# GpSimd's mixing steps spread over the quarters and tied to VectorE's steps, in a fused convolution with two expert layers

## The chip, the cores and the metric

The kernel runs on one core of one Trainium2 chip. The metric is the device time of one execution in microseconds; each version is run several times and the median is compared. Five engines of the core work here: PE (TensorE, matrix products, writes PSUM), DVE (VectorE), ACT (ScalarE), POOL (GpSimd, no access to PSUM) and SP (SyncE, which issues the DMAs). They are ordered against each other by semaphores only.

## The reference

`x` is 2 x 4096 x 192 (8192 tokens of 192 columns), everything in float32. Three parts follow each other.

```
w   = softmax(weight_gen, over k)                 # 7 weights per token and head, 8 heads of 24 columns
y0[s, h, :] = sum_k w[s, h, k] * x[s + k - 6, h, :]    # mixing over 7 tokens
u   = sigmoid(y0 @ w_gate) * (y0 @ w_val)         # 192 -> 1536
y   = u @ w_out1                                  # 1536 -> 192
h   = y @ w_in                                    # 192 -> 2048
g   = (a0 + a1 h + a2 h^2 + a3 h^3) / (1 + |b0| |h| + |b1| h^2 + 1e-6)
out = g @ w_out2                                  # 2048 -> 192
```

## The kernel before

The tokens are cut into 16 chunks of 512 (`NCH` = 16). Of the first layer a chunk has 12 units (128 of the 1536 columns each), of the second 16 (128 of the 2048). A loop over `k` of 73 steps, called quarters here, issues the work of every engine in an order written out by hand; a chunk of the first layer takes four quarters with three units each, and the second layer runs `OFF2` = 5 quarters behind with four units a quarter. In quarter `k`, `m = 3k`, `n = 4(k - 5)`, `p = n/2`.

PE's order within a quarter is the string `QUARTER`. "1" is `in1`: two products for a unit of the first layer (gate and value), each of them five matmuls (a float32 number is split into a high and a low part, so x and the weights come in parts). "2" is `in2`: one such product for a unit of the second layer. "a" and "b" are `out1` and `out2`: the unit's part in the layer's output, 8 matmul records each, added up in `acc1` and `acc2`. "a" lags one unit behind "1" (`A_LAG`), "b" eight units behind the quarter's first "2" (`B_LAG`). "X" transposes the mixed tokens of the next chunk (in the quarter with k % 4 = 3), "Y" transposes the first layer's output (k % 4 = 0). Products and transposes go into a ring of four PSUM banks; `wait_bank` makes PE wait until the bank used four places earlier is free: a gate product's by ACT's sigmoid, a value product's by `gated`, a "2" product's by `cubic`, a transpose's by `x_low` or `y_low`.

For a unit of the first layer ACT does `sigmoid` (L421) and DVE `gated` (L594). For a unit of the second ACT does `hidden` (L429, L430, L432: |b0 h|, h squared, a3 h + a2) and DVE `quadratic` (L601) and `cubic` (L607). These all read PSUM. For a pair of units DVE does `denominator` (L614); for four units ACT does `rsqrt` (L439) and `rsqrt_squared` (L446) on the denominator, which is a first estimate of its reciprocal; for a pair DVE does `newton_product` (L621), `reciprocal` (L628) and `quotient` (L637), after which "b" may run. These four DVE operations read two tensors in SBUF, 1024 elements a partition. Sigmoid and rsqrt need different tables of ACT, so there are two table loads a quarter.

A chunk's mixing is 13 steps (`mix`): a multiplication of the window by the weights of tap 0 into `mixed` (L519), then six times a multiplication into `prod` (L523) and an addition to `mixed` (L527). Chunk 0 is mixed by DVE, all others by GpSimd, which has nothing else to do: it begins a chunk when the transposes of the one before are done and its window is loaded, and runs through all 13 steps. `x_twice` (ACT, L396) then writes the last 64 columns a second time, since the transposes want 2 x 128 columns; `x_high` and `x_low` (ACT L404, L405; DVE L572, L575) split the transposed chunk. SP's order is `load_window(c)`, which waits for all 13 steps of chunk c - 1, and `store(c - 4)`. The first quarters also hold the softmax (L543 to L558) and the splitting of the weights (L564, L384).

Of the kernel before, what the change touches and what calls it, by code (L numbers as in the profile page):

```python
# [7 lines left out]
ALU = mybir.AluOpType  # L8
# [3 lines left out]
P = 128  # L12
T = 512
DA, DB = 128, 64
# [9 lines left out]
QUARTER = "12a212abbbXbYa12"  # L24
A_LAG = 1
B_LAG = 8
# [6 lines left out]
def moe_kernel(nc, x, weight_gen, w_gate, w_val, w_out1, w_in, w_out2, coef_a, coef_b, out):  # L33
# [34 lines left out]
    with ExitStack() as ctx:  # L68
        def sb(name, shape, dt=F32):
            return ctx.enter_context(nc.sbuf_tensor(name, shape, dt))  # L70
# [18 lines left out]

        window = sb("window", [P, WIN])  # L90
        mixw = sb("mixw", [P, CW])
        mixed = sb("mixed", [P, J, 2 * P])
# [3 lines left out]
        yt = [[sb(f"yt{b}_{n}", [P, T], F32R) for n in range(4)] for b in range(2)]  # L96
        ysb = sb("ysb", [P, J, 2 * P])
# [180 lines left out]
        def _(pe):  # L278
# [55 lines left out]
            def transposes(u, j, src):  # L334

                wait_bank(pe, u, j, 0)
                for n in range(J):
                    nc.tensor.transpose(bank(u, j, 0)[:, n * P:(n + 1) * P], src[:, n, 0:DA], ident[:, :])  # L338
                wait_bank(pe, u, j, 1)
                for n in range(J):  # L340
                    last = nc.tensor.transpose(bank(u, j, 1)[:, n * P:(n + 1) * P], src[:, n, DA:2 * P], ident[:, :])  # L341
                return last

            def x_transposes(j):
                pe.wait_ge(s_twice, j + 1)
                transposes("X", j, mixed).then_inc(s_xT, 1)

            def y_transposes(j):
                pe.wait_ge(s_ysb, j + 1)
                transposes("Y", j, ysb).then_inc(s_yT, 1)  # L350
# [29 lines left out]
        def _(act):  # L380
# [11 lines left out]
            def x_twice(j):  # L392
                if not 0 <= j < NCH:
                    return
                act.wait_ge(s_mix, MIXES * (j + 1))
                nc.scalar.copy(mixed[:, :, D:2 * P], mixed[:, :, DA:D]).then_inc(s_twice, 1)  # L396
# [77 lines left out]
            for k in range(NK):  # L474
                m, n, q = 3 * k, 4 * (k - OFF2), k - OFF2
                sigmoid(m)
                if k == 0:
                    split_high(4)
                    split_high(5)
                    exponential(1)  # L480
                    split_high(6)
                    split_high(7)
                hidden(n)
                if k % 4 == 0:
                    y_copy(k // 4 - 1)
                if k % 4 == 2:
                    x_twice((k + 1) // 4 + 1)
                hidden(n + 1)
                sigmoid(m + 1)
                if k == 1:  # L490
                    exponential(2)
                if k in (2, 3):
                    for c in range(3 * k + 2, 3 * k + 5):
                        split_high(c)
                rsqrt(q - 1)
                hidden(n + 2)
                rsqrt_squared(q - 1)
                if k % 4 == 3:
                    x_high(k // 4 + 1)
                if k % 4 == 0:  # L500
                    y_high(k // 4 - 1)
                sigmoid(m + 2)
                hidden(n + 3)
                if (k - OFF2) % 4 == 1:
                    z_copy((k - OFF2 - 1) // 4 - 1)

        def mix(eng, engine, c, k):
            base = MIXES * c
            m = (k + 1) // 2
            taken = window[:, m * D:m * D + J * D].rearrange("p (j h g) -> p j h g", h=H, g=G)  # L510
            total = mixed[:, :, 0:D]
            weights = softw[:, c * CW:(c + 1) * CW] if c < 2 else mixw[:, :]
            wk = weights.rearrange("p (j h k) -> p j h k", h=H, k=K)[:, :, :, m:m + 1].to_broadcast([P, J, H, G])
            if k == 0:
# [4 lines left out]
                engine.tensor_tensor(total.rearrange("p j (h g) -> p j h g", g=G), taken, wk,  # L519
                                     ALU.mult).then_inc(s_mix, 1)  # L520
            elif k % 2:
                wait(eng, s_mix, base + k if k > 1 else 0)
                engine.tensor_tensor(prod[:, :].rearrange("p (j h g) -> p j h g", h=H, g=G), taken, wk,  # L523
                                     ALU.mult).then_inc(s_mix, 1)
            else:
                eng.wait_ge(s_mix, base + k)
                engine.tensor_tensor(total, total, prod[:, :].rearrange("p (j d) -> p j d", d=D),  # L527
                                     ALU.add).then_inc(s_mix, 1)

        @block.vector  # L530
        def _(dve):
# [118 lines left out]
            for k in range(NK):  # L650
# [9 lines left out]
                quadratic(n)  # L660
                cubic(n)
                reciprocal(p - 3)
                denominator(p - 1)
# [12 lines left out]
                denominator(p)  # L676
                cubic(n + 1)
                quadratic(n + 2)
                cubic(n + 2)
                newton_product(p - 2)  # L680
                if k % 4 == 0:
                    y_low(k // 4 - 1)
                if k % 4 == 3:
                    x_low(k // 4 + 1)
                reciprocal(p - 2)
                gated(m + 2)
                quotient(p - 2)
                quadratic(n + 3)
                cubic(n + 3)
                newton_product(p - 1)  # L690

        @block.gpsimd
        def _(pool):
# [6 lines left out]
                                    base=0, pattern=[[-1, P]], channel_multiplier=1).then_inc(s_ident, 1)  # L700
            for c in range(1, NCH):
                for k in range(MIXES):
                    mix(pool, nc.gpsimd, c, k)
# [26 lines left out]
```

## Time and profile before

| | |
|---|---|
| median of 3 runs | 1509.95 us (1507.9 to 1510.64) |
| the profiled execution | 1511.6 us, of which the span of the trace is 1509.8 |
| mean granted clock of PE | 0.973 |
| PE busy | 1403.1 us, 93% of the span |
| DVE busy | 1277.7 us, 85% |
| ACT busy | 1047.7 us, 69% |
| GpSimd busy | 434.3 us, 29%, in 15 chunks |

All rows are of one profiled execution. A share is an average over three very different stages (the start, the steady quarters, the end without a first layer), so the stretches are read one by one. DVE's and PE's operations overlap a little at their ends: what one costs is read from start to start.

### The profile page before, as it was taken

Reading aid. Unit: us, or ns where it says so; the run is one execution under the profiler, and the core shown is the slowest. Engines: PE = TensorE matmul, PEld = TensorE weight load, DVE = VectorE, ACT = ScalarE, POOL = GpSimd, SP = SyncE. Lnnn points to the kernel's source line nnn. Section 1 sums busy time; section 2 is a strip of 40 time slices with the busy share of each in tenths; the row PEclk is TensorE's granted clock in tenths of the full one; section 3 lists DMA queues with packets and bytes.
Section 4 is the critical chain, followed back from the end, with each engine's and each line's share of the span. In section 5 each row is a group of like instructions: output and inputs, shape, how many; then the busy total and the mean of one; then the engine's idle time right before and its main releaser. Section 6 shows DMA issues by size and latency. Waiting matters only on the chain.

```text
span 1509.8 us, 18004 instructions
## 1 busy us (share of the span) xinstructions
PE 1403.1 (93%) x7040; PEld 1246.9 (83%) x7040; DVE 1277.7 (85%) x1327; ACT 1047.7 (69%) x1357; POOL 434.3 (29%) x204
## 2 busy tenths in 40 slices
PE   2689999999999999999999999999999999999886
PEld 1578888898988888888888888889888988898775
DVE  6556998989798898989889898988989898888896
ACT  2337777676777767677777767777776777777773
POOL 0632614306070340706134070512507052000000
PEclk9899999999999999999999999999999999999988
DMA  8410000000000000000000000000000000000000
GB/s 202 110 72 30 1 30 11 30 11 30 12 1 30 11 30 11 30 4 8 30 12 30 11 30 1 11 30 12 30 12 29 1 11 1 11 1 11 1 11 11
DMA packets 13102, 36.21 MB, mean 24 GB/s; under 512 B 1240, under 2 KB 6872, under 8 KB 12760
## 3 DMA queue, kind: packets, MB, share of 16 engines
q1 hardware_dynamic: 12952, 35.05, 7.6%
q8 instruction: 55, 0.90, 0.2%
q14 instruction: 31, 0.25, 0.1%
q0 software_dynamic: 64, 0.00, 0.0%
HBM read 27.16 MB, written 7.90 MB: 23 GB/s over the span
## 4 chain that ended last, share of the span: by engine, by line
PE 75%; DVE 15%; issue 5%; ACT 3%; DMA 1%; SPq 0%; DVEq 0%; ACTq 0%
PE ring L283 40%; PE acc L311 33%; DVE work L621 3%; DVE work L637 3%; DVE work L628 3%; DVE work L601 2%; PE ring L338 1%; ACT work L432 1%; DVE work L614 1%; PE ring L341 1%; DVE u L594 1%; ACT work L430 1%; ACT work L446 1%; DMA window<-in_x_dram 1%; DVE work L607 1%
## 5 line engine op out<-in xcount | busy, mean ns | idle before, releaser
L311 PE MATMUL acc<-out_w,work 128*128 128x192 f32 x2048 | 379.5, 345 | 52.4 <-DVE work L637 52.4
L311 PEld LDWEIGHTS acc<-out_w,work 128*128 128x128 f32 x2048 | 362.0, 203 | 59.2 <-DVE work L637 58.8
L283 PE MATMUL ring<-yt,in_w 128*128 128x512 f32 x1280 | 346.7, 402 | 0.9 <-DVE yt L586 0.9
L429 ACT ACTIVATE work<-ring,coef 128x512 f32<-128x512 f32 x256 | 176.2, 688 | 202.9 <-PE ring L283 189.5
L311 PE MATMUL acc<-out_w,u 128*128 128x192 f32 x1536 | 283.4, 328 | 17.1 <-DVE u L594 17.1
L283 PEld LDWEIGHTS ring<-yt,in_w 128*128 128x128 f32 x1280 | 238.5, 189 | 54.7 <-DVE work L607 4.0
L311 PEld LDWEIGHTS acc<-out_w,u 128*128 128x128 f32 x1536 | 259.2, 191 | 29.1 <-DVE u L594 18.2
L283 PE MATMUL ring<-xt,gate_w 128*128 128x512 f32 x960 | 268.5, 410 | 2.8 <-DVE xt L575 2.7
L283 PE MATMUL ring<-xt,val_w 128*128 128x512 f32 x960 | 256.7, 397 | 0.5 <-ACT u L421 0.5
L519 POOL TENSOR_TENSOR mixed<-window,mixw 128x768 f32<-128x768 f32 x14 | 30.2, 2158 | 767.9 <-PE ring L341 767.9
L601 DVE TENSOR_TENSOR work<-ring,work 128x512 f32<-128x512 f32 x256 | 175.6, 686 | 64.7 <-ACT work L432 64.7
L594 DVE TENSOR_TENSOR u<-ring,u 128x512 f32<-128x512 f32 x192 | 131.2, 684 | 115.6 <-PE ring L283 113.6
L283 PEld LDWEIGHTS ring<-xt,val_w 128*128 128x128 f32 x960 | 182.7, 191 | 44.4 <-ACT u L421 0.9
L283 PEld LDWEIGHTS ring<-xt,gate_w 128*128 128x128 f32 x960 | 182.3, 192 | 40.5 <-DVE xt L575 3.6
L621 DVE SCALAR_TENSOR_TENSOR work<-work 128x1024 f32<-128x1024 f32 x128 | 191.2, 1494 | 18.4 <-ACT work L446 18.4
L527 POOL TENSOR_TENSOR mixed<-mixed,prod 128x768 f32<-128x768 f32 x90 | 202.8, 2253 | 7.1
L432 ACT ACTIVATE work<-ring,coef 128x512 f32<-128x512 f32 x256 | 201.1, 786 | 0.0
L421 ACT ACTIVATE u<-ring 128x512 f32<-128x512 f32 x192 | 116.8, 609 | 119.2 <-PE ring L283 117.9
L637 DVE SCALAR_TENSOR_TENSOR work<-work,coef 128x1024 f32<-128x1024 f32 x128 | 197.5, 1543 | 0.2
L607 DVE SCALAR_TENSOR_TENSOR work<-work,coef,ring 128x512 f32<-128x512 f32 x256 | 190.8, 745 | 6.8
L523 POOL TENSOR_TENSOR prod<-window,mixw 128x768 f32<-128x768 f32 x84 | 187.8, 2236 | 5.5
L614 DVE SCALAR_TENSOR_TENSOR work<-work,coef 128x1024 f32<-128x1024 f32 x128 | 181.7, 1419 | 0.0
(57 smaller groups left out, 1012.7 us busy)
## 6 DMA issues: line engine op xcount, KB each, us to landing
window<-in_x_dram SPq DMA_DIRECT2D x14, 960.0 KB
out_dram<-zsb SPq DMA_DIRECT2D x16, 384.0 KB, 2.3
window<-in_x_dram SPq DMA_DIRECT2D x4, 472.5 KB
work<-in_weight_gen_dram SPq DMA_DIRECT2D x1, 1568.0 KB, 17.3
mix_weights<-work SPq DMA_DIRECT2D x1, 1568.0 KB, 5.1
mixw<-mix_weights SPq DMA_DIRECT2D x14, 112.0 KB
out_w<-in_moe_w_out_dram SPq DMA_DIRECT2D x1, 1536.0 KB, 23.5
out_w<-in_moe_w_out_dram SPq DMA_DIRECT2D x1, 1152.0 KB, 18.4
```

Source lines behind the costliest of these rows:

```text
L283: last = nc.tensor.matmul(dst[:, :], wt[:, c], xs[:, :], start=n == 0, stop=n == 4)
L311: last = nc.tensor.matmul(dst, src[:, n * P:(n + 1) * P], w[:, i, :], start=i == 0 and n % 2 == 0, stop=i == last_i and n % 2 == 1, skip_g ...
L429: nc.scalar.activation(den(n), h[:, :], ACT.Abs, scale=coef[:, 6:7])
L432: nc.scalar.activation(num(n), h[:, :], ACT.Identity, scale=coef[:, 3:4], bias=coef[:, 2:3]).then_inc(s_t1, 1)
L523: engine.tensor_tensor(prod[:, :].rearrange("p (j h g) -> p j h g", h=H, g=G), taken, wk, ALU.mult).then_inc(s_mix, 1)
L527: engine.tensor_tensor(total, total, prod[:, :].rearrange("p (j d) -> p j d", d=D), ALU.add).then_inc(s_mix, 1)
L594: nc.vector.tensor_tensor(u1[m % NU][:, :], bank("1", m, 1)[:, :], u1[m % NU][:, :], ALU.mult).then_inc(s_u, 1)
L601: nc.vector.tensor_tensor(num(n), bank("2", n)[:, :], num(n), ALU.mult).then_inc(s_t2, 1)
L607: nc.vector.scalar_tensor_tensor(out=num(n), in0=num(n), scalar=coef[:, 1:2], in1=bank("2", n)[:, :], op0=ALU.add, op1=ALU.mult).then_inc( ...
L614: nc.vector.scalar_tensor_tensor(out=den(2 * p, 2), in0=sqr(2 * p, 2), scalar=coef[:, 7:8], in1=den(2 * p, 2), op0=ALU.mult, op1=ALU.add). ...
L621: nc.vector.scalar_tensor_tensor(out=den(2 * p, 2), in0=den(2 * p, 2), scalar=Q_CONST, in1=sqr(2 * p, 2), op0=ALU.add, op1=ALU.mult).then_ ...
L637: nc.vector.scalar_tensor_tensor(out=num(2 * p, 2), in0=num(2 * p, 2), scalar=coef[:, 0:1], in1=den(2 * p, 2), op0=ALU.add, op1=ALU.mult). ...
```

## The change

GpSimd no longer runs a chunk's 13 steps in one go. `slot(c, k)` puts a wait in front of each: steps 0 to 3 belong to quarter 4c - 4, 4 to 7 to the next, 8 to 11 to the third, 12 to the fourth. Steps 0 and 3 of a quarter wait for its first quotient, step 1 for its second `gated`, step 2 for its second denominator. DVE's order is made for these places: newton, reciprocal and quotient of a pair now stand together, followed by `gated` and `quadratic`, and the second denominator is followed by PSUM operations. Both ACT and DVE now handle units n + 1 to n + 4 instead of n to n + 3 in a quarter. PE's order is another, with X one product before the quarter's end, and `B_LAG` is 9. `mixed` is narrower: the doubled columns have a tensor of their own, `x_pair`, which `x_twice` writes in full.

```diff
-QUARTER = "12a212abbbXbYa12"
+QUARTER = "21ab122bYbaab1X2"
 A_LAG = 1
-B_LAG = 8
+B_LAG = 9
...
-        mixed = sb("mixed", [P, J, 2 * P])
+        mixed = sb("mixed", [P, J, D])
...
+        x_pair = sb("x_pair", [P, J, 2, DB])
...
             def x_transposes(j):
                 pe.wait_ge(s_twice, j + 1)
-                transposes("X", j, mixed).then_inc(s_xT, 1)
+                transposes("X", j, lambda n: mixed[:, n, 0:DA], lambda n: x_pair[:, n, :, :].rearrange("p a d -> p (a d)")).then_inc(s_xT, 1)
...
                 act.wait_ge(s_mix, MIXES * (j + 1))
-                nc.scalar.copy(mixed[:, :, D:2 * P], mixed[:, :, DA:D]).then_inc(s_twice, 1)
+                wait(act, s_xT, j)
+                nc.scalar.copy(x_pair[:, :, :, :], mixed[:, :, DA:D].unsqueeze(2).to_broadcast([P, J, 2, DB])
+                               ).then_inc(s_twice, 1)
...
-                hidden(n)
                 if k % 4 == 0:
                     y_copy(k // 4 - 1)
-                if k % 4 == 2:
-                    x_twice((k + 1) // 4 + 1)
-                hidden(n + 1)
+                rsqrt(q - 1)
+                if (k - OFF2) % 4 == 2:
+                    z_copy((k - OFF2 - 2) // 4 - 1)
                 sigmoid(m + 1)
...
-                rsqrt(q - 1)
+                hidden(n + 1)
                 hidden(n + 2)
                 rsqrt_squared(q - 1)
+                if k % 4 == 0:
+                    y_high(k // 4 - 1)
+                if k % 4 == 3:
+                    x_twice(k // 4 + 1)
+                sigmoid(m + 2)
                 if k % 4 == 3:
                     x_high(k // 4 + 1)
-                if k % 4 == 0:
-                    y_high(k // 4 - 1)
-                sigmoid(m + 2)
                 hidden(n + 3)
-                if (k - OFF2) % 4 == 1:
-                    z_copy((k - OFF2 - 1) // 4 - 1)
+                hidden(n + 4)
...
-                quadratic(n)
-                cubic(n)
+                newton_product(p - 3)
                 reciprocal(p - 3)
-                denominator(p - 1)
                 quotient(p - 3)
                 gated(m + 1)
...
                 quadratic(n + 1)
                 denominator(p)
+                quadratic(n + 2)
                 cubic(n + 1)
-                quadratic(n + 2)
                 cubic(n + 2)
                 newton_product(p - 2)
                 if k % 4 == 0:
                     y_low(k // 4 - 1)
+                reciprocal(p - 2)
+                quotient(p - 2)
+                gated(m + 2)
                 if k % 4 == 3:
                     x_low(k // 4 + 1)
-                reciprocal(p - 2)
-                gated(m + 2)
-                quotient(p - 2)
                 quadratic(n + 3)
+                denominator(p + 1)
                 cubic(n + 3)
-                newton_product(p - 1)
+                quadratic(n + 4)
+                cubic(n + 4)
...
+            def slot(c, k):
+                quarter = 4 * c - 4 + k // 4
+                if k % 4 in (0, 3):
+                    wait(pool, s_g, 2 * (quarter - OFF2 - 2) + 2)
+                elif k % 4 == 1:
+                    wait(pool, s_u, 3 * quarter + 2)
+                elif k % 4 == 2:
+                    wait(pool, s_q, 2 * (quarter - OFF2) + 2)
+
             for c in range(1, NCH):
                 for k in range(MIXES):
+                    slot(c, k)
                     mix(pool, nc.gpsimd, c, k)
```

## Rows read from the trace of the kernel before

**Rows 1.** Windows: length; busy us (instructions) of PE, PEld, DVE, ACT, POOL; clock, DMA, GB/s.

```profile
502.60:591.60 89.00, 86.64 (x442) 77.27 (x441) 78.25 (x81) 65.06 (x85) 29.45 (x13) 0.98 0.05 18
591.60:679.50 87.90, 85.21 (x442) 75.57 (x441) 78.01 (x81) 64.93 (x85) 29.45 (x13) 1.00 0.05 17
...
1319.00:1402.70 83.70, 83.70 (x434) 74.91 (x433) 68.84 (x79) 63.48 (x81) 0.00 (x0) 1.00 0.02 6
1402.70:1509.80 107.10, 78.40 (x342) 70.88 (x340) 90.86 (x95) 65.17 (x82) 0.00 (x0) 0.85 0.02 8
```

**Rows 2.** Waits of PE from 140 to 1400 us: total us, times, longest.

```profile
PE acc L311 <- DVE work L637: 29.1, 13, 2.4
```

**Rows 3.** Timeline of PE, a quarter without mixing: start us, us, what.

```profile
563.29 1.45 PE L283 MATMUL ring<-xt,gate_w 128*128 128x512 f32 x5
...
577.64 5.36 PE L311 MATMUL acc<-out_w,work 128*128 128x192 f32 x32
582.84 1.46 PE L311 MATMUL acc<-out_w,u 128*128 128x192 f32 x8
584.00 1.45 PE L283 MATMUL ring<-xt,gate_w 128*128 128x512 f32 x5
```

**Rows 4.** Timeline of PE: gate products after X or 12 units, and a stall.

```profile
163.98 1.46 PE L283 MATMUL ring<-xt,gate_w 128*128 128x512 f32 x5
...
625.21 2.87 PE L311 MATMUL acc<-out_w,work 128*128 128x192 f32 x16 [2.32 <-DVE work L637]
...
1315.54 1.46 PE L283 MATMUL ring<-xt,gate_w 128*128 128x512 f32 x5
...
1399.26 1.45 PE L283 MATMUL ring<-xt,gate_w 128*128 128x512 f32 x5
```

**Rows 5.** Timeline of GpSimd in a burst.

```profile
612.59 1.83 POOL L527 TENSOR_TENSOR mixed<-mixed,prod 128x768 f32<-128x768 f32 x1
614.50 2.41 POOL L523 TENSOR_TENSOR prod<-window,mixw 128x768 f32<-128x768 f32 x1
```

**Rows 6.** Timeline of DVE beside it.

```profile
612.68 2.83 DVE L621 SCALAR_TENSOR_TENSOR work<-work 128x1024 f32<-128x1024 f32 x1
615.43 0.68 DVE L594 TENSOR_TENSOR u<-ring,u 128x512 f32<-128x512 f32 x1
```

**Rows 7.** Timeline of GpSimd while DVE waits for PE.

```profile
54.92 1.54 POOL L523 TENSOR_TENSOR prod<-window,work 128x768 f32<-128x768 f32 x1
56.54 1.84 POOL L527 TENSOR_TENSOR mixed<-mixed,prod 128x768 f32<-128x768 f32 x1
```

**Rows 8.** Timeline of DVE in quarters without mixing.

```profile
582.27 1.23 DVE L621 SCALAR_TENSOR_TENSOR work<-work 128x1024 f32<-128x1024 f32 x1 [0.32 <-ACT work L446]
583.53 1.23 DVE L628 SCALAR_TENSOR_TENSOR work<-work 128x1024 f32<-128x1024 f32 x1
...
596.91 1.28 DVE L637 SCALAR_TENSOR_TENSOR work<-work,coef 128x1024 f32<-128x1024 f32 x1
598.11 0.68 DVE L594 TENSOR_TENSOR u<-ring,u 128x512 f32<-128x512 f32 x1
598.71 0.68 DVE L601 TENSOR_TENSOR work<-ring,work 128x512 f32<-128x512 f32 x1
...
600.50 0.74 DVE L607 SCALAR_TENSOR_TENSOR work<-work,coef,ring 128x512 f32<-128x512 f32 x1
```

**Rows 9.** Timeline of ACT.

```profile
575.41 1.28 ACT L439 ACT_TABLE_LOAD   x1
576.70 2.00 ACT L439 ACTIVATE work<-work,qconst 128x2048 f32<-128x2048 f32 x1
...
580.32 1.91 ACT L446 ACTIVATE work<-work 128x2048 f32<-128x2048 f32 x1
```

**Rows 10.** Timeline of PE near the end: the last product 2.

```profile
1481.44 1.51 PE L283 MATMUL ring<-yt,in_w 128*128 128x512 f32 x5
```

**Rows 11.** Timeline of DVE near the end: the last quotient.

```profile
1500.61 1.28 DVE L637 SCALAR_TENSOR_TENSOR work<-work,coef 128x1024 f32<-128x1024 f32 x1
```

More of the change, by code:

```diff
@@ L332, in out2, with transposes @@
                 second_product(acc2, out2_w, num(n), i, F2 - 1).then_inc(s_out2, 1)
-            def transposes(u, j, src):
+            def transposes(u, j, upper, lower):
                 wait_bank(pe, u, j, 0)
                 for n in range(J):
-                    nc.tensor.transpose(bank(u, j, 0)[:, n * P:(n + 1) * P], src[:, n, 0:DA], ident[:, :])
+                    nc.tensor.transpose(bank(u, j, 0)[:, n * P:(n + 1) * P], upper(n), ident[:, :])
                 wait_bank(pe, u, j, 1)
                 for n in range(J):
-                    last = nc.tensor.transpose(bank(u, j, 1)[:, n * P:(n + 1) * P], src[:, n, DA:2 * P], ident[:, :])
+                    last = nc.tensor.transpose(bank(u, j, 1)[:, n * P:(n + 1) * P], lower(n), ident[:, :])
                 return last
@@ L345, in x_transposes @@
                 pe.wait_ge(s_twice, j + 1)
-                transposes("X", j, mixed).then_inc(s_xT, 1)
+                transposes("X", j, lambda n: mixed[:, n, 0:DA], lambda n: x_pair[:, n, :, :].rearrange("p a d -> p (a d)")).then_inc(s_xT, 1)
             def y_transposes(j):
                 pe.wait_ge(s_ysb, j + 1)
-                transposes("Y", j, ysb).then_inc(s_yT, 1)
+                transposes("Y", j, lambda n: ysb[:, n, 0:DA], lambda n: ysb[:, n, DA:2 * P]).then_inc(s_yT, 1)
             pe.wait_ge(s_ident, 2)
@@ L509, in mix @@
             m = (k + 1) // 2
-            taken = window[:, m * D:m * D + J * D].rearrange("p (j h g) -> p j h g", h=H, g=G)
-            total = mixed[:, :, 0:D]
+            taken = window[:, m * D:m * D + J * D].rearrange("p (n g) -> p n g", g=G)
             weights = softw[:, c * CW:(c + 1) * CW] if c < 2 else mixw[:, :]
-            wk = weights.rearrange("p (j h k) -> p j h k", h=H, k=K)[:, :, :, m:m + 1].to_broadcast([P, J, H, G])
+            wk = weights.rearrange("p (n k) -> p n k", k=K)[:, :, m:m + 1].to_broadcast([P, J * H, G])
             if k == 0:
@@ L518, in mix @@
                 wait(eng, s_xT, c)
-                engine.tensor_tensor(total.rearrange("p j (h g) -> p j h g", g=G), taken, wk,
+                engine.tensor_tensor(mixed[:, :, :].rearrange("p j (h g) -> p (j h) g", g=G), taken, wk,
                                      ALU.mult).then_inc(s_mix, 1)
@@ L522, in mix @@
                 wait(eng, s_mix, base + k if k > 1 else 0)
-                engine.tensor_tensor(prod[:, :].rearrange("p (j h g) -> p j h g", h=H, g=G), taken, wk,
+                engine.tensor_tensor(prod[:, :].rearrange("p (n g) -> p n g", g=G), taken, wk,
                                      ALU.mult).then_inc(s_mix, 1)
@@ L526, in mix @@
                 eng.wait_ge(s_mix, base + k)
-                engine.tensor_tensor(total, total, prod[:, :].rearrange("p (j d) -> p j d", d=D),
-                                     ALU.add).then_inc(s_mix, 1)
+                flat = mixed[:, :, :].rearrange("p j d -> p (j d)")
+                engine.tensor_tensor(flat, flat, prod[:, :], ALU.add).then_inc(s_mix, 1)
         @block.vector
```

## The prediction

> **What bounds the kernel now.** I read the page first: PE is busy for 93% of the span, DVE for 85%, ACT for 69%. That names PE, but not why 7% is missing. The busy times by stretch tell it [rows 1]. From 1319.0 to 1402.7 GpSimd is idle, and PE is busy for all of 83.70 us at full clock. In 502.6 to 591.6, a chunk of the same work with one burst of GpSimd steps in it, the chunk takes 89.0 us instead. In the last 107 us PE is busy for 78 only and DVE for 91: there DVE is the bound.
>
> One undisturbed quarter is 20.71 us, from the gate product at 563.29 to the one at 584.00 [rows 3]. Four units of `out2` take 582.84 - 577.64 = 5.20, so 1.30 a unit. A quarter has 7 such units (a, b) and 10 products of five matmuls: (20.71 - 7 x 1.30) / 10 = 1.16 a product. The mixing-free chunk takes 1399.26 - 1315.54 = 83.72 [rows 4], which is 4 x 20.71 + 0.88: the 0.88 is one pair of transposes (Y). A chunk with X and Y should thus take 4 x 20.71 + 2 x 0.88 = 84.6. The 13 chunks between 163.98 and 1315.54 take 1151.56, so 88.6 each: 4.0 us too much, 52 us in all. The waits of PE from 140 to 1400 us name one cause, 13 times, once a chunk: the quotient L637, 29.1 us [rows 2]. The rest of the 52 is the refilling of the pipeline after each of these waits and a lower clock: the chunk with a mean granted clock of 0.98 took 89.0, its neighbour at 1.00 took 87.9 [rows 1]. A stall goes with all it brings behind it.
>
> **Why the quotient is late.** GpSimd's step at 612.59 ends at 614.42. VectorE's L621, which begins at 612.68, ends only at 615.51, 1.09 us after it. GpSimd's next step is called at 614.50, but ends at 616.91, 1.40 after L621 [rows 5, 6]. So the two engines take turns: a GpSimd step and a VectorE operation with two SBUF inputs hold something exclusively for their whole length. In the same burst L594, which reads PSUM, takes its ordinary 0.68. The holds are 1.40 for a multiplication and some 1.7 for an addition (its 1.83 less the start-up), 13 x 1.54 = 20 us a chunk. The burst puts nearly all of them within 29 us, 1.4 quarters.
>
> **VectorE's slack.** From start to start: quotient 1.20, gated and quadratic 0.60, cubic 0.67 (0.74 less the same overlap), newton and reciprocal 1.26 where the next operation needs the result [rows 8], a denominator as a quotient. A quarter of the new order: 3 x 0.60 + 4 x 0.60 + 4 x 0.67 + 2 x 1.20 + 4 x 1.26 + 2 x 1.20 = 16.7. PE gives it 20.71, so 4 us are free. In a burst of 1.4 quarters 5.6 us are free, while five or six holds cost 8 to 9: the missing 3 us is the stall of today.
>
> **The changed quarter, step by step** (0 is PE's start of its first 2; n, m, p as in the code). PE starts: 2 0; 1 1.16; a 3.48; b 4.78; 1 6.08; 2 8.40; 2 9.57; b 10.7; (Y); b 12.0; a 13.3; a 14.6; b 15.9; 1 17.2; (X); 2 19.6. ACT's rsqrt takes 2.00 less an overlap of some 0.09, `hidden` the 1.72 from then to 580.32, a table load 1.28 [rows 9]. ACT: the last two `hidden` of the quarter before until 3.7, sigmoid 4.3, rsqrt 7.5, sigmoid 9.5, `hidden(n+1)` and `hidden(n+2)` until 13.3, rsqrt squared 15.2, sigmoid 18.6 to 19.2. DVE: quadratic and denominator until 3.9, cubic, quadratic, cubic until 6.0, gated 6.6, the triple newton, reciprocal, quotient until 10.3, gated 10.9, quadratic(n+1) from 11.7 (it waits for ACT), denominator 12.3 to 13.5, quadratic and two cubics until 15.4, the second triple until 19.1, gated at 19.8.
>
> PE's deadlines against this: the bank of 2(n) is wanted at 7.2 and free at 6.0; that of 2(n-1) wanted at 6.1, free at 4.6; gated(m) wanted at 9.6, done 6.6; `out2(n-6)` at 15.9 wants the quotient of 10.3, which in the old order is the wait of [rows 2]; `hidden(n+2)` wants the same quotient at 11.6. None has less than 1.1 us to spare, GpSimd not yet counted.
>
> **GpSimd in it.** Each chunk has 13 steps, now 4, 4, 4 and 1 in its quarters. Alone a step takes 1.62 (multiplication) or 1.92 (addition) to the next [rows 7]. Steps 2 and 3 start behind the denominator (3.9) and run until 7.3; PSUM operations fill 3.9 to 6.6; the newton step waits 0.7. Steps 0 and 1 start behind the quotient (11.0 with that delay) and run until 14.3; the denominator, at 12.3, waits for step 0, up to 0.4, and step 1 then waits for it and ends before the next newton. So 1.1 us are lost where each wait for ACT or PE (0.8, 0.7 and 2 us) absorbs it, and no deadline is touched: `hidden(n+2)` still has 0.6 us on its quotient. Bounds: 0, and all 3.25 holds at 1.54, that is 5.0 (a rival below). I take 1.1. The waits of GpSimd itself hold up nothing but its own queue: `x_twice` wants step 12 at 15.2, done at 13. SP's next window load hangs on step 12 and has a whole quarter before step 0. `x_twice` now copies 512 elements instead of 256, which costs some 0.2 us on an ACT that is 76% busy in [rows 1]; the row of `mixed` becomes contiguous, which I cost at nothing: GpSimd has 11 of 21 us free.
>
> **X later in the quarter.** The X transposes now stand one product before the quarter's end. From their end to x_low's, two casts (0.6 each, a third of a `hidden`) and one subtraction (0.68) pass with hand-overs, some 2.1 us; the two products 2 in front of the next gate product cover 2.3. That is the tightest place: 0.2 us. At 0.15 to 0.3 us missing in 13 chunks it costs 2 to 4 us; I put in 2.
>
> **The sum, against this execution's own time** (span 1509.8, outside it 1.8).
> - Quarters 8 to 59: 52 x 20.71 + 26 x 0.88 = 1099.8 instead of 1151.6, plus 2 for X: -50.
> - Start: before quarter 5 there are no products 2 behind X, so chunk 1's x_low is waited for in full, +2. Chunk 1's steps 9 to 12 now wait for gated(7) and fall on the softmax and the weight splits, which read two SBUF tensors: 2 to 3 holds of 1.54, less one saved earlier, +3. One `out2` less in quarter 7, -1.3. The filling of the pipeline, 0 to 1.5. Together +4 (bounds 0 and +8).
> - Quarters 60 to 63: 0.
> - End, 107.1 us today: DVE-bound, no GpSimd in it. From the last product 2 (1481.44) to the last quotient (1500.61 + 1.28) are 20.4 us [rows 10, 11]. The new order puts denominator(127) at once behind the last quadratic, and the pair 125 beside the last rsqrt: 1.5 for the product, 1.9 `hidden`, 1.8, rsqrt and its square 3.9 (beside pair 125), two triples 7.4, so 17: -3. The extra `out2` lies in a PE that waits. Together -3 (bounds -6 and +3).
>
> For the chained operations, first the row: newton to reciprocal is 1.26 where they are neighbours [rows 8], against 1.14 to 1.20 unchained; two more such pairs a quarter in five DVE-bound quarters make about +1, which is in the end's bounds. The Trainium skill, "VectorE: DVE Perf Modes", section "The DRAIN you can't avoid", has it that a semaphore between chained operations costs nothing extra; by it that +1 would be 0. This trace does not agree.
>
> 1509.8 - 50 + 4 - 3 = 1461 for the span, 1463 with what lies outside. The profiled run (1511.6) stands 1.65 above the median of the three runs, so 1461; I say 1460.
>
> **Rivals.**
> (a) Part of the stall stays: x_low, or the Y quarter (1.2 us more for DVE, 1.1 more for ACT), makes PE wait 1 to 2 us once a chunk, and each wait may cost another 1 us at the lower clock: 13 x (1 to 3) = 13 to 39, so 1473 to 1499, say 1485. For it: margins of 0.2 and about 1 us. Against it: the free 2 us before the next quadratic.
> (b) Slower: the steps do not fit behind the denominator and the quotient but make a two-SBUF operation wait each time. Then DVE's quarter is 16.7 + 5.0 = 21.7 and every quarter is DVE-bound: 1.0 x 52, plus 2.4 - 1.8 = 0.6 in 13 chunks: 60, so 1520. It decides from 4.0 us of holds a quarter on and loses against today from about 4.9. For it: two steps in a row are 3.3 us long, while the room behind the quotient is 1.4. Against it: step 1 falls where four PSUM operations follow.
> (c) No change: the stalls have another root than the burst, so the order only moves them: 1510. Against it stands the chunk without a burst [rows 1].
>
> **Chances.** The forecast (1450 to 1472) 0.70; (a) 0.19; (b) 0.08; (c) 0.03. The range is 1450 to 1488: below it the best start and end (-7), above it most of (a). What a measurement here can tell from no change is 0.2%, 3 us. Faster 0.89, same 0.03, slower 0.08.
>
> **What would show it.** Right: chunks of 84.6 in quarters 8 to 59, PE busy for all of them, clock 1.00; no PE wait on the quotient before 1350 us; GpSimd steps in twos, L594 and L601 beside them at 0.68; newton longest at some 2 us; 2 to 3 us wait before the first gate product of chunk 1. Wrong: a PE wait on x_low or on a bank in each chunk (a), or steady quarters longer than 20.71 with DVE at 95% or more (b).

## The result, and the profile after

The changed kernel takes 1457.17 us in the median of four runs (1456.45 to 1458.5), the kernel before, run beside it, 1509.7. The ratio is 0.9654, 95% interval 0.9638 to 0.9671. The forecast was 1460, range 1450 to 1488. The profiled execution has a span of 1454.7 us, 55.1 less than before, at a mean granted clock of 0.987 instead of 0.973.

The sum of the prediction gave 1461 for the span, so the terms together are 6.3 us off. The median is off by only 2.8, and that is luck: the execution profiled before lies 1.65 above its median, this one 0.7 below, and the forecast was rounded down by 1.

First the busy times by stretch, cut where the quarters 8 and 60 begin and where quarter 64 ends up (columns as in [rows 1]); under it the only wait of PE from 140 to 1345 us, to be held against [rows 2].

```profile
171.70:1271.20 1099.50, 1099.50 (x5720) 983.62 (x5720) 957.95 (x1041) 843.67 (x1093) 303.31 (x169) 1.00 0.06 17
1271.20:1355.00 83.80, 83.80 (x434) 74.93 (x433) 69.83 (x80) 63.70 (x82) 0.00 (x0) 1.00 0.02 6
1355.00:1454.70 99.70, 71.85 (x350) 62.91 (x348) 89.10 (x94) 64.99 (x82) 0.00 (x0) 0.95 0.02 8
```

```profile
PE ring L284 <- DVE u L596: 1.2, 1, 1.2
```

In the 1099.50 us of quarters 8 to 59 PE is busy for 1099.50 us, at full clock. The 13 waits on the quotient are gone (the one wait left lies at 153 us, in the filling of the pipeline). So the four stretches compare like this; the first two of before follow from [rows 4] (quarter 8 begins three products, 3.49 us, behind the gate product at 163.98):

| stretch | before | forecast | after |
|---|---|---|---|
| start, to quarter 8 | 167.5 | 171.5 | 171.7 |
| quarters 8 to 59 | 1151.6 | 1101.8 | 1099.5 |
| quarters 60 to 63 | 83.7 | 83.7 | 83.8 |
| end | 107.1 | 104.1 | 99.7 |

PE's timeline around X, the narrow place, and from one gate product (612.71) to that of the next quarter (633.43):

```profile
593.14 0.60 PE L342 MATMUL ring<-ident,x_pair 128*128 128x128 f32 x4
593.50 2.57 PE L284 MATMUL ring<-yt,in_w 128*128 128x512 f32 x10
595.90 1.32 PE L284 MATMUL ring<-xt,gate_w 128*128 128x512 f32 x5
...
612.71 1.46 PE L284 MATMUL ring<-xt,gate_w 128*128 128x512 f32 x5
...
633.43 1.45 PE L284 MATMUL ring<-xt,gate_w 128*128 128x512 f32 x5
```

612.71 to 633.43 is 20.72, a quarter as before in [rows 3]. Behind X (593.14) two products cover the way to the new chunk's first gate product at 595.90; its row shows no wait. `x_twice` on ACT, which reads the chunk's step 12, waits for nothing either.

DVE and GpSimd in the same stretch (GpSimd's rows second; the first two of DVE are newton and reciprocal unhindered) answer to [rows 5] and [rows 6]:

```profile
589.20 1.21 DVE L623 SCALAR_TENSOR_TENSOR work<-work 128x1024 f32<-128x1024 f32 x1
590.44 1.22 DVE L630 SCALAR_TENSOR_TENSOR work<-work 128x1024 f32<-128x1024 f32 x1
...
622.85 2.11 DVE L623 SCALAR_TENSOR_TENSOR work<-work 128x1024 f32<-128x1024 f32 x1
...
627.46 0.68 DVE L596 TENSOR_TENSOR u<-ring,u 128x512 f32<-128x512 f32 x1
628.06 0.68 DVE L603 TENSOR_TENSOR work<-ring,work 128x512 f32<-128x512 f32 x1
628.66 1.87 DVE L616 SCALAR_TENSOR_TENSOR work<-work,coef 128x1024 f32<-128x1024 f32 x1
...
605.13 1.54 POOL L521 TENSOR_TENSOR mixed<-window,mixw 128x768 f32<-128x768 f32 x1 [18.85 <-DVE work L639]
...
622.33 1.55 POOL L525 TENSOR_TENSOR prod<-window,mixw 128x768 f32<-128x768 f32 x1
627.62 1.82 POOL L530 TENSOR_TENSOR mixed<-mixed,prod 128x768 f32<-128x768 f32 x1 [3.74 <-DVE work L639]
629.58 2.34 POOL L525 TENSOR_TENSOR prod<-window,mixw 128x768 f32<-128x768 f32 x1
```

The step of 622.33 runs until 623.88, and newton (L623), begun at 622.85, takes 2.11 instead of 1.22: it had to wait for the rest of one hold, 0.9 us. The step of 627.62 begins with `gated` (L596) and lies beside it and `quadratic` (L603), both at 0.68; the denominator (L616) at 628.66 waits for its end at 629.44 and takes 1.87 instead of 1.28. The next step (629.58) waits in turn and takes 2.34 instead of 1.54. Where a quarter's steps find only PSUM operations a multiplication takes 1.54 (605.13) and an addition 1.82 (627.62), as in [rows 7]; the new, contiguous row of `mixed` makes no difference there. In the 13 chunks the holds cost DVE 0.96 us a quarter (how this is measured stands at the end of the experiments). They come out of DVE's waits (for ACT 115 us of `quadratic`'s between 180 and 1340 us instead of 147 with thin steps, for PE 1 instead of 20), and nothing of them reaches PE.

### The profile page after: what moved, and what is told of

Same layout as the page of the kernel before. It is cut to its first block, busy times and chain, and to the rows that moved or that the text cites. A ratio compares the mean times of both kernels' runs of the same rounds, so it can differ in the third digit from the quotient of the medians.

```text
span 1454.7 us, 18169 instructions
## 1 busy us (share of the span) xinstructions
PE 1375.1 (95%) x7040; PEld 1224.0 (84%) x7040; DVE 1221.6 (84%) x1327; ACT 1047.2 (72%) x1357; POOL 356.3 (24%) x204
## 4 chain that ended last, share of the span: by engine, by line
PE 88%; DVE 8%; ACT 2%; issue 1%; DMA 1%; SPq 0%; ACTq 0%; DVEq 0%
PE ring L284 48%; PE acc L312 37%; DVE work L630 1%; DVE work L639 1%; DVE work L623 1%; PE ring L339 1%; DVE work L609 1%; PE ring L342 1%; DVE work L603 1%; DMA window<-in_x_dram 1%; DVE work L616 1%; DVE mixed L530 0%; DVE prod L525 0%; DVE in_w L566 0%; ACT work L433 0%
## 5 line engine op out<-in xcount | busy, mean ns | idle before, releaser
L312 PE MATMUL acc<-out_w,work 128*128 128x192 f32 x2048 | 371.4, 329 | 20.9 <-DVE work L639 17.8
L312 PEld LDWEIGHTS acc<-out_w,work 128*128 128x128 f32 x2048 | 342.4, 192 | 30.0 <-DVE work L639 21.1
L284 PE MATMUL ring<-yt,in_w 128*128 128x512 f32 x1280 | 321.8, 397 | 3.4 <-DVE work L609 1.7
L530 POOL TENSOR_TENSOR mixed<-mixed,prod 128x768 f32<-128x768 f32 x90 | 164.5, 1828 | 562.6 <-DVE work L616 412.2
L312 PE MATMUL acc<-out_w,u 128*128 128x192 f32 x1536 | 275.7, 330 | 19.5 <-DVE u L596 19.5
L603 DVE TENSOR_TENSOR work<-ring,work 128x512 f32<-128x512 f32 x256 | 175.4, 685 | 130.1 <-ACT work L435 128.4
L284 PE MATMUL ring<-xt,gate_w 128*128 128x512 f32 x960 | 274.6, 416 | 4.6 <-DVE xt L577 4.6
L623 DVE SCALAR_TENSOR_TENSOR work<-work 128x1024 f32<-128x1024 f32 x128 | 191.4, 1495 | 0.0
L609 DVE SCALAR_TENSOR_TENSOR work<-work,coef,ring 128x512 f32<-128x512 f32 x256 | 184.4, 740 | 2.3
L616 DVE SCALAR_TENSOR_TENSOR work<-work,coef 128x1024 f32<-128x1024 f32 x128 | 184.1, 1438 | 0.0
L596 DVE TENSOR_TENSOR u<-ring,u 128x512 f32<-128x512 f32 x192 | 131.6, 686 | 60.7 <-PE ring L284 42.3
L639 DVE SCALAR_TENSOR_TENSOR work<-work,coef 128x1024 f32<-128x1024 f32 x128 | 164.5, 1285 | 4.5
L630 DVE SCALAR_TENSOR_TENSOR work<-work 128x1024 f32<-128x1024 f32 x128 | 156.7, 1224 | 3.9
L525 POOL TENSOR_TENSOR prod<-window,mixw 128x768 f32<-128x768 f32 x84 | 150.6, 1793 | 28.6 <-DVE u L596 19.1
## 6 DMA issues: line engine op xcount, KB each, us to landing
work<-in_weight_gen_dram SPq DMA_DIRECT2D x1, 1568.0 KB, 16.5
```

Of the source, the lines that this page charges most:

```text
L284: last = nc.tensor.matmul(dst[:, :], wt[:, c], xs[:, :], start=n == 0, stop=n == 4)
L312: last = nc.tensor.matmul(dst, src[:, n * P:(n + 1) * P], w[:, i, :], start=i == 0 and n % 2 == 0, stop=i == last_i and n % 2 == 1, skip_g ...
L525: engine.tensor_tensor(prod[:, :].rearrange("p (n g) -> p n g", g=G), taken, wk, ALU.mult).then_inc(s_mix, 1)
L530: engine.tensor_tensor(flat, flat, prod[:, :], ALU.add).then_inc(s_mix, 1)
L603: nc.vector.tensor_tensor(num(n), bank("2", n)[:, :], num(n), ALU.mult).then_inc(s_t2, 1)
L609: nc.vector.scalar_tensor_tensor(out=num(n), in0=num(n), scalar=coef[:, 1:2], in1=bank("2", n)[:, :], op0=ALU.add, op1=ALU.mult).then_inc( ...
```

## The experiments

All ratios are to the kernel before, run beside the experiment on the same chip; its medians were 1509.1 to 1509.7, so a difference of an experiment to the changed kernel is known to about 1 us.

**Is it the slots or the new order?** One line is taken out of the changed kernel:

```diff
             for c in range(1, NCH):
                 for k in range(MIXES):
-                    slot(c, k)
                     mix(pool, nc.gpsimd, c, k)
```

> The changed kernel without the waits of slot: GpSimd runs a chunk's 13 steps in one go again, in the new order of PE, ACT and DVE. Theory A (spreading is what removes the stall): 13 x 1.54 = 20 us of holds fall on 1.4 quarters with 1.4 x 4 = 5.6 us to spare; the new order lets DVE be 1.2 us late before a bank is wanted, so 1.5 to 3.5 us of PE wait come back in each of 13 chunks: 1477 to 1503 us, with a wait of PE on quotient, cubic or gated once a chunk. Theory B (the order alone did it, for the quotient now has 5 us to spare before its b): no PE wait in the steady quarters, 1452 to 1460 us. Under both the start loses some 3 us of contention with the softmax.

Measured: 1510.11 us, ratio 1.0006 (0.9993 to 1.0019). PE's timeline in the Y quarter, then DVE's rows ahead of the wait:

```profile
628.27 0.60 PE L339 MATMUL ring<-ident,ysb 128*128 128x128 f32 x4
631.59 0.66 PE L342 MATMUL ring<-ident,ysb 128*128 128x128 f32 x4 [2.72 <-DVE u L596]
...
623.84 1.87 DVE L623 SCALAR_TENSOR_TENSOR work<-work 128x1024 f32<-128x1024 f32 x1
625.74 2.45 DVE L630 SCALAR_TENSOR_TENSOR work<-work 128x1024 f32<-128x1024 f32 x1
628.22 2.71 DVE L639 SCALAR_TENSOR_TENSOR work<-work,coef 128x1024 f32<-128x1024 f32 x1
```

The order alone is worth nothing in the sum: its shorter end (185.8 us behind the X of quarter 59, as in the changed kernel) is used up by stalls a little dearer than before. A stall comes back once a chunk, as theory A has it, but on `gated` and not on the quotient: the three chained operations from 623.84 on lose 3.3 us together to the holds, `gated` (L596) stands behind them, and the bank of the second Y transpose (L342) waits for it, 2.7 us in each of 13 chunks. The size was forecast too low (1477 to 1503). The waits, 2.9 us a chunk in all, lie within the 1.5 to 3.5 expected; what I had not counted is what a wait brings behind it. Two neighbouring chunks, in the columns of [rows 1]:

```profile
524.89:614.03 89.14, 86.44 (x441) 77.04 (x440) 77.34 (x80) 65.01 (x84) 28.69 (x13) 0.98 0.05 17
614.03:702.48 88.45, 85.23 (x441) 75.48 (x440) 77.67 (x80) 65.12 (x84) 28.72 (x13) 1.00 0.05 18
```

Both hold the wait of 2.7, the second one also a wait of 0.5; but at its lower mean clock PE is busy 1.2 us longer in the first, for the same matmuls. The mean of the 13 chunks is 88.89, 4.3 above 84.60.

**Are the holds the cause in the old kernel?** GpSimd's steps 1 to 12 of each chunk are cut to 24 columns of one token; most of the mixing is left out.

```diff
+            slim = c > 0 and k > 0
+            if slim:
+                taken, wk, total = taken[:, 0:1, 0:1, :], wk[:, 0:1, 0:1, :], mixed[:, 0:1, 0:G]
+            part = prod[:, 0:G] if slim else prod[:, :]
```

> The kernel before with GpSimd's steps 1 to 12 of every chunk on 24 columns of one token instead of 768 elements (most of the mixing is left out; number and order of the instructions stay). Theory A (holds of GpSimd make the stall): the 13 waits on L637 vanish and chunks take 84.6 us, so 1510 - 52, and 1 to 3 less in the start: 1453 to 1459 us. Theory C (the old order of the engines stalls once a chunk by itself, at the Y quarter): 1490 us or more, with the waits on L637 still there.

Measured: 1458.8 us, ratio 0.967 (0.9651 to 0.9689). PE has no wait at all from 172 to 1345 us, and the X transposes come 84.60 us apart:

```profile
245.14 0.60 PE L338 MATMUL ring<-ident,mixed 128*128 128x128 f32 x4
...
329.74 0.60 PE L338 MATMUL ring<-ident,mixed 128*128 128x128 f32 x4
```

So the old order does not stall by itself, which was the rival (c) and theory C. The 52 us of the steady stretch were GpSimd's holds: the 13 chunks take 1099.8 instead of 1151.6.

**The same in the changed kernel.**

> The changed kernel with the same thin steps 1 to 12 (most of the mixing is left out). If the holds that are left (newton up to 2.1 us) cost nothing in the steady quarters, only the start can gain: 1451 to 1456 us. If they cost something that the trace hides, the steady quarters get shorter than 20.71 + 0.88 where due, and the time falls below 1450.

Measured: 1451.6 us, ratio 0.9622 (0.9603 to 0.9641). The X transposes come 84.60 us apart here as well (165.16, 249.76, 334.36), with the first 4.5 us earlier than the 169.65 of the changed kernel. What is left of the holds costs nothing in the steady quarters; the 4 to 5 us lie in the start.

**Does the place count, or only the spreading?**

```diff
                 quarter = 4 * c - 4 + k // 4
-                if k % 4 in (0, 3):
+                if c > 2 and k % 4 in (0, 1):
+                    wait(pool, s_u, 3 * quarter + 1)
+                elif c > 2:
+                    wait(pool, s_t, quarter - OFF2)
+                elif k % 4 in (0, 3):
```

> The changed kernel with other places for GpSimd's steps from chunk 3 on: steps 0 and 1 of a quarter are released by gated(m), steps 2 and 3 by rsqrt_squared, each just ahead of newton, reciprocal and quotient, which read two SBUF tensors. As evenly spread as before, 4, 4, 4, 1. Theory A' (the place counts as well as the spreading): up to four holds of 1.54 a quarter, 16.7 + 6.2 = 22.9 us of DVE against 20.7 in three of four quarters, so 1 to 2 us a quarter: 1490 to 1540 us, PE waiting for DVE. Theory D (spreading alone is enough, any place will do): 1457 to 1465 us.

Measured: 1503.62 us, ratio 0.9963 (0.995 to 0.9976). PE's waits in the steady quarters, and the two stretched operations of DVE:

```profile
PE ring L284 <- DVE u L596: 26.0, 26, 1.0
PE ring L342 <- DVE u L596: 9.4, 13, 0.8
...
620.85 2.46 DVE L630 SCALAR_TENSOR_TENSOR work<-work 128x1024 f32<-128x1024 f32 x1
623.35 2.45 DVE L639 SCALAR_TENSOR_TENSOR work<-work,coef 128x1024 f32<-128x1024 f32 x1
```

The steps are spread as evenly as before and nearly the whole gain is gone: the place counts. A chunk takes 346.77 - 258.65 = 88.12 us. The waits, 1.0 in two quarters and 0.7 in the Y quarter, again cost more than their length, 3.5 against 2.7. The clock stays at 1.00 all through these 13 chunks, so it has no part in this. The time is less than in the rival (b) of the prediction (1520), for DVE lost 15 us a chunk to the holds and not 20: in the 13 chunks it is busy for 1103.96 us against 909.29 with thin steps.

**Does it need the new order?** The kernel before gets the waits of `slot`; `x_twice` moves to the quarter in which step 12 comes.

```diff
-                if k % 4 == 2:
-                    x_twice((k + 1) // 4 + 1)
...
                 rsqrt(q - 1)
+                if k % 4 == 3:
+                    x_twice(k // 4 + 1)
                 hidden(n + 2)
...
+                    slot(c, k)
                     mix(pool, nc.gpsimd, c, k)
```

> The kernel before, with the waits of slot in front of GpSimd's steps (x_twice moved to the quarter with k % 4 = 3, between rsqrt and hidden(n + 2), for step 12 comes then). Orders of PE, ACT and DVE, B_LAG and mixed are the old ones. There the second denominator of the slot comes in the next quarter, directly ahead of the quotient, so steps 2 and 3 make the quotient wait, and b wants it with little to spare. Theory A (the order is needed for these places): a wait of 0.3 to 1.5 us on the quotient in most quarters with four steps, 1470 to 1500 us. Theory D (the spreading is enough in either order): 1455 to 1465 us.

Measured: 1520.4 us, ratio 1.0075 (1.0061 to 1.0089): 0.75% slower than before, outside both ranges. GpSimd's last three steps of a chunk, and PE behind them:

```profile
602.12 2.81 POOL L527 TENSOR_TENSOR mixed<-mixed,prod 128x768 f32<-128x768 f32 x1 [10.97 <-DVE work L614]
605.06 2.34 POOL L523 TENSOR_TENSOR prod<-window,mixw 128x768 f32<-128x768 f32 x1
607.55 1.80 POOL L527 TENSOR_TENSOR mixed<-mixed,prod 128x768 f32<-128x768 f32 x1
...
609.84 1.12 PE L338 MATMUL ring<-ident,mixed 128*128 128x128 f32 x4 [2.40 <-ACT mixed L396]
```

No wait on the quotient is left, but steps 10 and 11 come one quarter late, since the old order has its second denominator there, and push step 12 to 607.55 to 609.35. ACT stands still at `x_twice` until then (DVE waits 4.9 us for ACT's next result), PE waits 2.4 us for it, and a chunk takes 609.84 - 521.08 = 88.76. A single wait set to the wrong place, that of every second pair of steps, undid the whole. So the place was mended:

```diff
                 elif k % 4 == 2:
-                    wait(pool, s_q, 2 * (quarter - OFF2) + 2)
+                    wait(pool, s_q, 2 * (quarter - OFF2) + 1)
```

> e7 with one wait changed: steps 2 and 3 wait for the first denominator of their own quarter instead of the one that the old order puts into the next quarter. In e7 PE waited on nothing but x_twice, 2.4 us in each of 13 chunks, since step 12 queued behind steps 10 and 11. Theory A' (only that queueing made e7 slow, and the old order otherwise takes spread steps): step 12 starts at the quotient, the wait is gone, 1455 to 1465 us. Theory E (the old order cannot take them: four steps in a row behind one quotient, 3 holds on denominator, newton and reciprocal): waits on quotient or gated of 0.5 us and more, 1475 to 1510 us.

Measured: 1462.65 us, ratio 0.9689 (0.9675 to 0.9704). The steady stretch of this kernel:

```profile
171.70:1271.20 1099.50, 1099.50 (x5721) 984.99 (x5720) 1008.30 (x1041) 842.70 (x1092) 346.76 (x169) 1.00 0.06 17
```

PE is as full as in the changed kernel, although DVE is busy for 1008 us instead of 958. In the steady quarters the old order takes the spread steps just as well; theory E falls. What DVE loses to the holds, from its busy time in the 13 chunks between the X of quarter 7 and that of quarter 59, against the kernel with thin steps in the same order (912.31 old, 909.29 new; the first step of a chunk is whole there, so these are lower bounds):

| kernel | DVE busy | lost, us a chunk | PE idle, us a chunk |
|---|---|---|---|
| changed kernel | 958.99 | 3.8 | 0 |
| old order, spread (this one) | 1008.60 | 7.4 | 0 |
| changed kernel without slots | 1006.92 | 7.5 | 2.9 |
| kernel before | 1015.51 | 7.9 | 2.4 |
| two-SBUF places | 1103.96 | 15.0 | 2.7 |

With 7.4 us spread over a chunk nothing is lost, with 7.5 in one burst 4.3 us: this pair shows most plainly what the spreading does. The new places do something else, they halve the loss, and here that half was not needed. What the old order lacks is the end: X of quarter 7 at 164.63 puts quarter 8, 6.83 us behind it in this order, at 171.5, and 1461.8 - 171.5 - 1099.6 - 83.7 = 107.0 is the end of [rows 1] again, where the changed kernel has 99.7.

**What does the lag do?** The changed kernel with `B_LAG` 8:

> The changed kernel with B_LAG = 8 instead of 9. out2(n - 6) then stands at 12.0 us of the quarter instead of 15.9, against a quotient at 10.3 to 11.0. If that margin is real, nothing changes in the steady quarters and the end is the same within 1 us: 1456 to 1459 us. If the lag of 9 carries part of the gain (the quotient later than I worked out), PE waits on L639 in many quarters: 1465 us or more.

Measured: 1544.36 us, ratio 1.0232 (1.0218 to 1.0246), in the range of the second theory, but by neither one's cause. One row of PE tells it:

```profile
607.28 2.93 PE L312 MATMUL acc<-out_w,work 128*128 128x192 f32 x8 [3.37 <-ACT zsb L466]
```

It is `z_copy` (L466), 3.4 us in each of 13 chunks: with lag 8 the first b of the quarter opens the next chunk and wants `acc2` free at 4.8 us, while ACT copies it behind rsqrt, at 7.5. The eight matmuls after it take 2.93 instead of 1.46, half the speed. `z_copy` moved to the front of its quarter, with lag 8:

> e8 (B_LAG 8) with z_copy moved to the front of its quarter on ACT, ahead of sigmoid(m), still one quarter after the last out2 of its chunk. In e8 PE waited 3.4 us for z_copy in each of 13 chunks. Theory A (lag 8 failed through z_copy alone, the quotient has its margin): z_copy is over at 4.4 us, before the first b at 4.8, and the time is that of the changed kernel within 2 us, 1456 to 1459. Theory B (the lag itself is needed): PE waits on L639 in many quarters, 1465 us or more.

Measured: 1460.72 us, ratio 0.9676 (0.9662 to 0.9691). The steady quarters are full again (1099.50 of 1099.50) and none waits on the quotient. The margin that I gave the quotient is real, and the lag of 9 serves `z_copy`. The time is 3.6 us above the changed kernel's, 1.6 more than I allowed; the spans (1459.5 against 1454.7) differ by 2.9 in the start (X of quarter 7 at 172.53 instead of 169.65, of which one more `out2` is 1.3) and by 2.0 behind the X of quarter 59 (187.29 us instead of 185.28). So the lag of 9 has a share in the shorter end.

**How narrow is the place behind X?** One more subtraction of x_low's size ahead of it, from chunk 2 on:

```diff
                 dve.wait_ge(s_xh, 2 * j + 1)
+                if j > 1:
+                    nc.vector.tensor_tensor(spare[:, :], bank("X", j, 0)[:, :], dst[0][:, :].bitcast(F32),
+                                            ALU.subtract).then_inc(s_spare, 1)
```

> The changed kernel with one more subtraction of x_low's size (into a spare tensor) ahead of x_low from chunk 2 on: 0.6 us more between the X transposes and the gate product that wants them, 14 times. If the margin there is the 0.2 us of the prediction: PE waits 0.4 to 0.5 us in each of 14 chunks, 6 to 7 us more than the changed kernel, 1463 to 1464 us. If the place has more room, 1457 to 1458 us; if a short wait also costs clock, 1470 us and more.

Measured: 1467.47 us, ratio 0.9723 (0.9707 to 0.974), 10 above the changed kernel, between the expected ranges.

```profile
514.27 1.39 PE L286 MATMUL ring<-xt,gate_w 128*128 128x512 f32 x5 [0.43 <-DVE xt L584]
```

The wait is 0.43 for 0.60 more work: the margin was 0.17 us. But a chunk grows by 0.68 (254.68 to 339.94 is 85.26), so again a wait costs more than its length, here at a clock that stays at 1.00.

**The start, and a better version.** The one edit, then what was expected:

```diff
-                    slot(c, k)
+                    if c > 1:
+                        slot(c, k)
```

> The changed kernel, but chunk 1's 13 steps run without the waits of slot, all others with them. In the changed kernel steps 9 to 12 of chunk 1 fall on L560 and L566 (three of L566 take 5.76 us there, 2.93 before) and the PE wait that follows ends on them. Free, they are over before: L566 gets 2.8 us shorter, while L548 gets its 1.3 us back (4.78 against 3.47). Theory A (the start's contention moved, term +3 of the sum): 1.3 to 3 us faster than the changed kernel, 1454 to 1456 us. Theory B (PE's waits in the start are set by the softmax and the loads alone): 1457 us, no change.

Measured: 1453.4 us, ratio 0.9636 (0.9623 to 0.9649), a little more gain than expected; span 1451.6 against 1454.7. DVE in the start, first of the changed kernel, then of this one:

```profile
60.12 3.47 DVE L548 TENSOR_TENSOR work<-work,ysb 128x3136 f32<-128x3136 f32 x1
...
84.35 5.76 DVE L566 TENSOR_TENSOR in_w<-work,in_w 128x768 fp32r<-128x768 f32 x3
...
90.76 2.93 PE L312 MATMUL acc<-out_w,u 128*128 128x192 f32 x8 [6.73 <-DVE u L596]
...
105.02 1.45 PE L284 MATMUL ring<-xt,gate_w 128*128 128x512 f32 x5 [2.09 <-DVE xt L577]
```

```profile
61.55 3.71 DVE L548 TENSOR_TENSOR work<-work,ysb 128x3136 f32<-128x3136 f32 x1
...
86.00 2.93 DVE L566 TENSOR_TENSOR in_w<-work,in_w 128x768 fp32r<-128x768 f32 x3
...
89.58 1.57 PE L312 MATMUL acc<-out_w,u 128*128 128x192 f32 x8 [3.74 <-DVE u L596]
...
101.35 2.41 PE L284 MATMUL ring<-xt,gate_w 128*128 128x512 f32 x5 [2.09 <-DVE xt L577]
```

The three splits (L566) are back at 2.93 from 5.76 and PE waits 3.74 instead of 6.73, as it did in the kernel before. L548 did not go back to the 4.78 expected; it took 3.71. Then X one unit earlier in quarter 3 alone:

```diff
+EARLY_X = "21ab122bYbaabX12"
...
-                for u in QUARTER:
+                for u in (EARLY_X if k == 3 else QUARTER):
...
+                if k == 3:
+                    x_high(1)
                 sigmoid(m + 2)
...
+                if k == 3:
+                    x_low(1)
                 gated(m + 2)
```

> e5 (chunk 1's steps free) and, in quarter 3 alone, X one unit earlier (ahead of the third 1), with x_high ahead of that unit's sigmoid and x_low ahead of its gated. PE's 2.1 us wait before chunk 1's first gate product, with the 1.0 us that this product then takes longer at the lower clock, lies behind the unit's 2.3 us. If so, 2 to 3 us less than e5: 1450 to 1452 us. If the transposes only wait elsewhere (for x_twice or a bank), no change: 1453 to 1454 us.

Measured: 1449.6 us, ratio 0.9607 (0.9593 to 0.9621), below the changed kernel's interval. The wait of 2.09 us is gone: chunk 1's first gate product, at 102.87 now, waits for nothing. The trace doesn't show the gain, though. The profiled execution is the slowest of the four (1452.72 against 1448.92 to 1449.63) and reaches the X of quarter 7 at 165.82, against 165.93 with chunk 1 free alone, since its first X came 0.8 us later (27.91) and its wait at 74.62 is 1.1 longer. By the medians this is the fastest version of the study.

## Why the prediction was right

**The turn-taking and the stall, right.** That GpSimd's steps and DVE's two-SBUF operations hold each other for their full length, and that PSUM operations do not take part, is in the rows of both kernels. That this makes the 52 us is shown by the thinned steps (1458.8) and by the burst put back (1510.1).

**Quarters 8 to 59: -52.1 measured, -50 forecast.** The 2 us put in for x_low were not needed; its margin, given as 0.2, measures 0.17. The forecast of 1.1 us lost in a quarter measures 0.96. DVE's loss in the burst of the kernel before, put at "five or six holds" or 8 to 9 us, measures 7.9 a chunk. The other end of the bounds, 5.0 a quarter, was not reached: the two-SBUF places gave 3.7 (15.0 a chunk) and 1503.6 us.

**The start: +4.2 measured, +4 forecast.** The wait for x_low is 2.09 (forecast 2). The splits lose 2.8, the subtraction L548 wins 1.3 (3.47 instead of 4.78) and the last split wins 1.3 as well (2.40 instead of 3.66), since chunk 2's steps no longer fall on it; the second win was not in the sum. The free chunk 1 wins back 3.7 (X of quarter 7 at 165.93). The old order with slots has a start of 171.5 as well, with the wait behind the splits (6.72) and without the one for x_low, so the two starts are equal in length and not in all their terms.

**The end: -7.4 measured, -3 forecast.** This term was mis-sized, just outside its own bounds (-6 and +3). I counted only the chain from the last product 2 to the last quotient's end, and put it at 17 us (its terms add up to 16.5) instead of 20.4. It measures 18.9:

```profile
1429.25 2.11 PE L284 MATMUL ring<-yt,in_w 128*128 128x512 f32 x5
...
1446.91 1.28 DVE L639 SCALAR_TENSOR_TENSOR work<-work,coef 128x1024 f32<-128x1024 f32 x1
```

So the chain gave 1.5 and not 3.4; the other 5.9 lie where I had put nothing: 4.5 ahead of that product (74.25 us from the stretch's beginning instead of 78.74) and 1.4 behind the quotient. DVE's waits in the whole end, before and after:

```profile
DVE work L621 <- ACT work L446: 4.4, 6, 2.8
DVE work L601 <- ACT work L432: 2.3, 7, 1.2
DVE u L594 <- PE ring L283: 1.9, 1, 1.9
DVE yt L583 <- ACT yt L413: 0.5, 1, 0.5
```

```profile
DVE work L603 <- ACT work L435: 3.1, 5, 2.4
```

That is 9.1 us before and 3.1 after. The longest one before, 2.8 us for the last rsqrt squared, was in front of the last two pairs; now pair 125 runs meanwhile, as the prediction had it. The quarters bound by DVE repeat in 15.64 us before and in 15.24 after:

```profile
1429.83 4.55 PE L311 MATMUL acc<-out_w,work 128*128 128x192 f32 x16 [3.44 <-DVE work L637]
...
1445.47 5.48 PE L311 MATMUL acc<-out_w,work 128*128 128x192 f32 x16 [3.83 <-DVE work L637]
```

```profile
1411.73 1.57 PE L312 MATMUL acc<-out_w,work 128*128 128x192 f32 x8 [0.17 <-DVE work L639]
...
1426.97 2.73 PE L312 MATMUL acc<-out_w,work 128*128 128x192 f32 x8 [4.68 <-DVE work L639]
```

The 1.4 behind the last quotient is the way from its end to the span's: 7.9 us before (1509.8 less the 1501.9 of [rows 11]) and 6.5 now. The old order with spread steps kept its 107 us, so the 7 us belong to the new order, the lag of 9 included (with lag 8 some 2 of them are gone), and the 52 to the steps.

**The chained operations.** Newton to reciprocal is 1.24 apart in the changed kernel (589.20 to 590.44), about as in [rows 8], against 1.13 from newton to a `y_low` that does not need its result (611.51 to 612.64). The Trainium skill ("VectorE: DVE Perf Modes", section "The DRAIN you can't avoid") reports eight copies that took the same time with a semaphore after each as with one at the end. The chained pairs here are 0.11 dearer all the same; no run has such a pair without its semaphore, so what costs the 0.11 stays open. The DVE-bound end became shorter nonetheless, by the waits that went.

**Where I was wrong around it.** Both experiments by which I wanted to weigh the order and the lag failed on another queue than the one that I watched: `x_twice` behind a late step 12, `z_copy` behind rsqrt. Neither was in the expectation, and both cost more than the change had won.

## What to carry to other kernels

Before an engine's side work is spread, find which of the main engine's operations it blocks and tie each step to the end of such an operation where others follow; even distances on the wrong operations gave nearly nothing here. But look at the slack too: the plain spread in the old order cost DVE twice as much as the chosen places and PE nothing. Count a wait of PE not by its length but by what the repeated stretch grows: it was 1.3 to 1.8 times as much. After each shift by one unit or one quarter, look up every consumer of the moved step on every engine, the copies that free a buffer first.

## What the runs showed of the hardware

The two-SBUF operations of DVE and GpSimd's tensor operations exclude each other in turns for whole instructions, 1.4 to 1.7 us a turn; an operation of DVE with one PSUM input ran at 0.68 beside them in every row read. The same holds the other way round for a long operation of DVE: beside L548 (3.47 us from 60.12 on) a multiplication of GpSimd, called at 60.38, took 4.61 and ended 1.40 behind it.

PE's idle time and what it costs a chunk (length above 84.60), means of the 13 chunks between the X of quarter 7 and that of quarter 59, and the mean granted clock of this stretch:

| kernel | PE idle, us a chunk | chunk, us | cost, us | clock |
|---|---|---|---|---|
| x_low longer | 0.46 | 85.29 | 0.7 | 1.00 |
| two-SBUF places, 3 waits a chunk | 2.7 | 88.10 | 3.5 | 1.00 |
| kernel before | 2.4 | 88.58 | 4.0 | 0.99 |
| old order, late step 12 | 2.4 | 88.64 | 4.0 | 0.98 |
| changed kernel without slots | 2.9 | 88.89 | 4.3 | 0.99 |
| lag 8 | 3.4 | 90.48 | 5.9 | 0.97 |

The part of the cost beyond the idle time is PE being busy longer for the same matmuls. At full clock it is about 0.25 us a wait (x_low longer: 0.24; two-SBUF places: 0.8 for three). The rest goes with the lower clock: behind the 3.4 us of lag 8 PE has a granted clock of 0.50 from 607.3 to 610.0, its lower level of 1.2 GHz. In single chunks both levels of cost stand side by side: without slots 88.45 at 1.00 and 89.14 at 0.98. The two-SBUF places have as much idle time a chunk as the kernels that wait once, in three pieces of at most 1.0 us, and their mean clock reads 1.00.
